# Attention in front of the feed forward, or in pieces between its products: a three-stage kernel on one core

## The chip, the core and the metric

The kernel runs on one core of a Trainium2 chip. The core has TensorE (PE, matrix products, with its weight loads as PEld), VectorE (DVE), ScalarE (ACT), GpSimd (POOL) and SyncE (SP, here only issuing DMAs). Each engine works off its own instructions in order; they meet only in semaphores. TensorE writes to PSUM (eight banks of 128 x 512 floats), the others read it from there and keep their results in SBUF. The metric is the device time of one execution in microseconds. A median of 3 runs of the kernel before is 901.97 us (901.59 to 902.38).

## The reference

```python
def _attn_ref(q, k, v):                  # (4, 8, 576, 64) each
    scores = scale * np.matmul(q, k.transpose(0, 1, 3, 2))
    mask = (rel >= 0) & (rel < 64)       # causal, a window of 64
    scores = np.where(mask, scores, -1000000000.0)
    attn = softmax(scores)               # max, exp, sum + 1e-9
    return np.matmul(attn, v)

def _moe_ref(x, w_in, w_out):            # x: 2304 x 512, w_in: 512 x 2048
    h = x @ w_in
    return (h - np.tanh(h)) @ w_out

def _moe2_ref(x, expert_emb, tau, w1, w2):
    # each row's best expert of 8 by cosine, its softmax weight as a gate;
    # out[mask] = gate * (np.maximum(x[mask] @ w1[e], 0) @ w2[e])
```

The three follow one another: attention's output, 2304 rows of 512, is the x of the feed forward, whose output is routed to the experts. All is float32. A product of the second and third stage is made of three products of "high" and "low" parts in a rounded type (float32r): high x high, high x low, low x high.

## The kernel before, in words

**Attention.** The sequence has 36 blocks of 64 positions (9 in each of 4 batches). A *group* is 3 such blocks of one pair of heads; there are 48 groups, each for one pair (4) and one *window* of 192 positions (12). Per group PE turns q and k (L1003, 3 transposes), DVE copies them out of PSUM (L721, L723: "evacuate"), PE makes the scores (L1012, 3 products in 6 records), DVE masks and takes the maximum (L728), ACT takes exp (L536), DVE inverts the sums (L749, L754), POOL scales (L416), PE turns the result (L1021), ACT copies it (L544), PE multiplies by v (L1032), ACT copies the output to xT (L553). DVE also copies v shifted by one block (L738). The engines run these steps skewed over the groups: in one round of PE stand transposes of group j, scores of j-1, turn of j-5 and attend of j-7. A hardware loop goes over the batches. POOL splits w_in meanwhile (L428, L431) from a staging buffer.

**Feed forward.** Only when all 48 groups are done does PE begin it. The rows are 6 blocks of 384 (two windows with all four pairs: 8 groups). A *step* (n, c) is one of 16 chunks of 128 hidden columns: `first_product(n, c)` (12 products of 384 columns), tanh on ACT (L581), h - tanh on DVE (L796), the high part on ACT (L585), the low part on DVE (L798), and, two steps later, `second_product` (9 products of 512 columns into three PSUM banks). PE's order is

```python
def step(n, c):
    first_product(n, c)
    if c >= 2:
        second_product(n, c - 2)
    ...
    if not (isinstance(n, int) and n == 0):
        after_block(n - 1, c)
```

where `after_block` routes the rows of the block before: transposes of x2 (L1097), logits (L1107), ranks, and small DVE work. In block 0 POOL splits w_out.

**Experts.** The rest, from the last product of the feed forward on, works through 25 tiles of rows with their expert's weights. The change doesn't touch it, only the buffers' places.

The order on every engine is written out by hand; SP issues the loads in the order of its own program, each waiting for the buffer that it fills.

Of the kernel before, what the change touches and what calls it, by code (L numbers as in the profile page):

```python
# [6 lines left out]
F32R = mybir.dt.float32r  # L7
# [4 lines left out]
ds = bass.ds  # L12
# [5 lines left out]
HEAD = 9  # L18
# [16 lines left out]
def build(nc, q, k, v, w_in, w_out, emb, tau, w1, w2, out):  # L35
# [15 lines left out]
    NT = T // P  # L51

# [9 lines left out]
    with ExitStack() as ctx:  # L62
# [37 lines left out]
        changes = sb("changes", [P, NTILE + 1])  # L100

        phase1 = ctx.enter_context(ExitStack())
        xT = sb("xT", [P, NW, PAIRS, GT], scope=phase1)
        win_h = sb("win_h", [P, KC, F], F32R, phase1)
        win_l = sb("win_l", [P, KC, F], F32R, phase1)
        attn = ExitStack()

        vw = [sb(f"vw{i}", [P, NB + 1, 2, D], scope=attn) for i in range(PAIRS)]
        qbd = [sb(f"qbd{i}", [P, NB, 2, WINDOW], scope=attn) for i in range(2)]
        sm = [sb(f"sm{i}", [P, GB, P], scope=attn) for i in range(4)]  # L110
        pn = [sb(f"pn{i}", [P, GB, P], scope=attn) for i in range(4)]
# [3 lines left out]
        plain_ones = sb("plain_ones", [P, P], scope=attn)  # L115
        plain_tri = sb("plain_tri", [P, P], scope=attn)
# [5 lines left out]
        stage = sb("stage", [P, 2, F], scope=attn)  # L122

        kT = [sb(f"kT{i}", [P, NB + 1, WINDOW], scope=attn) for i in range(2)]
        qk = [sb(f"qk{i}", [P, NB, 2, D], scope=attn) for i in range(2)]
        attn.close()
        wout_h = sb("wout_h", [P, FC, DM], F32R, phase1)
        wout_l = sb("wout_l", [P, FC, DM], F32R, phase1)
        xh = sb("xh", [P, KC, 2, 2, GT], F32R, phase1)
        xl = sb("xl", [P, KC, 2, 2, GT], F32R, phase1)  # L130
        early = ExitStack()
# [3 lines left out]
        zrow = sb("zrow", [1, DM], scope=early)  # L135
        en1 = sb("en1", [E, 3], scope=early)
        enroot = sb("enroot", [E, 1], scope=early)
        early.close()
        gf_tile = sb("gf", [P, 2, TB], scope=phase1)
        gf = [gf_tile[:, i, :] for i in range(2)]  # L140
        gh = [sb(f"gh{i}", [P, TB], F32R, phase1) for i in range(2)]
        gl = [sb(f"gl{i}", [P, TB], F32R, phase1) for i in range(2)]
# [3 lines left out]
        x2T, junk = (xT[:].rearrange("p w k t -> p (w k t)")[:, i * BANK:(i + 1) * BANK] for i in (0, 1))  # L146
# [38 lines left out]
        first_loaded, v_shifted = sem("first_loaded"), sem("v_shifted")  # L185
        qk_loaded, v_loaded = sems("qk_loaded", 2), sems("v_loaded", PAIRS)
        win_loaded, win_split = sem("win_loaded"), sem("win_split")
        win_high = sem("win_high")
        qk_transposed, qk_evacuated = sem("qk_transposed"), sem("qk_evacuated")
        scored, maxed, exped = sem("scored"), sem("maxed"), sem("exped")  # L190
        sum_padded, inverted, normed = sem("sum_padded"), sem("inverted"), sem("normed")
        p_transposed, pT_copied, attended, x_copied = sem("p_transposed"), sem("pT_copied"), sem("attended"), sem("x_copied")
        wout_loaded = sems("wout_loaded", ST)
# [28 lines left out]
        psT, psS, psP, psO = ([grouped(2 * n + i) for i in range(2)] for n in range(4))  # L222
        psH = [banks[:, i, 0:TB] for i in (0, 1)]
        acc = [banks[:, 2 + i, :] for i in range(ST)]
        psX = banks[:, 5, :]
        psX_last = [banks[:, i, :] for i in (5, 2, 3)]
        psJ = banks[:, 0, :]
        psL = banks[:, 6, 0:ST * E].rearrange("p (s e) -> p s e", s=ST)
        psR = banks[:, 7, 0:ST * E].rearrange("p (s e) -> p s e", s=ST)
        psN = banks[:, 7, 0:E]  # L230
# [15 lines left out]
        def attention(eng, step):  # L246

            for j in range(HEAD):
                step(0, j)
            with eng.Fori(0, B - 1) as b:  # L250
                for j in range(HEAD, HEAD + GPB):
                    step(b, j)
            for j in range(HEAD, GPB + 7):
                step(B - 1, j)

        def feed_forward(eng, step):

            for c in range(FC):
                step(0, c)
            with eng.Fori(1, NBLK - 1) as n:  # L260
                for c in range(FC):
                    step(n, c)
            for c in range(FC):
                step(NBLK - 1, c)
# [28 lines left out]

        block = ctx.enter_context(nc.Block())

        @block.sync
        def _(sp):
            def load_qk(b, hp):
                i = hp % 2

                wait(sp, qk_transposed, 0 if isinstance(b, int) and PAIRS * b + hp < 2 else GPB * b + GP * (hp - 1))
                for blocks, to in ((q_blocks, qk[i][0:WINDOW]), (k_blocks, qk[i][WINDOW:P])):
                    for h in range(2):
                        sp.dma_start(to[:, :, h, :], blocks[:, ds((2 * PAIRS * b + 2 * hp + h) * NB, NB), :]).then_inc(qk_loaded[i], 16)

            def load_v(b, hp):
                if not isinstance(b, int) or b > 0:

                    sp.wait_ge(attended, GPB * b + GP * (hp + 1 - PAIRS))
                for h in range(2):  # L310
                    sp.dma_start(vw[hp][0:WINDOW, 1:, h, :], v_blocks[:, ds((2 * PAIRS * b + 2 * hp + h) * NB, NB), :]).then_inc(v_loaded[hp], 16)

            def load_w_in(row):
                sp.dma_start(stage[:, ds(row % 2, 1), :], win_rows[:, ds(row, 1), :]).then_inc(win_loaded, 16)

            def load_batch(b, more=True):

                for hp in range(PAIRS):
                    load_v(b, hp)
# [958 lines left out]
```

## Time and profile before

| | |
|---|---|
| median of 3 runs | 901.97 us |
| span of the profiled execution, first to last instruction | 897.8 us |
| PE busy | 826.8 us (92%) |
| DVE busy | 431.8 us (48%) |
| ACT busy | 368.3 us (41%) |
| POOL busy | 188.9 us (21%) |

The profile gives the profiled execution's time as its span only; what lies around the span is the difference to the median, 901.97 - 897.8 = 4.2 us. Busy shares are means over three stages with different limits, so they have to be read stage by stage. The trace has one line per instruction or run of like instructions: start in us, length in us, engine, line, what is written from what, how often, and in brackets how long the engine had stood idle and who ended that.

### The profile page before, as it was taken

How to read it: one execution, taken by the hardware profiler on the slowest of the kernel's cores; microseconds unless marked ns; L12 is line 12 of the kernel's file. 1: busy time of each engine (PE TensorE's matmuls, PEld its weight loads, DVE VectorE, ACT ScalarE, POOL GpSimd, SP SyncE). 2: the span in 40 equal slices, each digit the busy share in tenths (PEclk: the TensorE clock that was granted, in tenths of full speed). 3: DMA queues.
4: the chain of work that ended last, by engine and by line, in shares of the span. 5: the costliest groups of instructions: out<-in, count | busy, mean ns of one | idle time of the engine just before them, and what ended most of it. 6: DMA issues, size and time to landing. Idle time of an engine off the chain costs nothing. (4 is left out here: it accounts for less than half of the span.)

```text
span 897.8 us, 16837 instructions
## 1 busy us (share of the span) xinstructions
PE 826.8 (92%) x4496; PEld 726.4 (81%) x4497; DVE 431.8 (48%) x1214; ACT 368.3 (41%) x888; POOL 188.9 (21%) x224
## 2 busy tenths in 40 slices
PE   5988878999999999999999999758999999999992
PEld 4877777999999999999999999637888888888871
DVE  6999996332343343344334334465435152355312
ACT  3888886233222223223223222506435262455423
POOL 3755557900001001001001001021111111111111
PEclk9999999999999999999999999869999999999996
DMA  9966841300000000000000320006634251655110
GB/s 166 185 147 142 133 92 36 118 1 32 5 1 1 35 0 0 35 0 0 35 0 0 128 95 1 36 25 223 224 120 141 79 193 41 224 216 212 64 36 25
DMA packets 80463, 72.87 MB, mean 81 GB/s; under 512 B 60364, under 2 KB 60497, under 8 KB 79906
## 3 DMA queue, kind: packets, MB, share of 16 engines
q1 hardware_dynamic: 75794, 61.00, 24.3%
q0 software_dynamic: 4624, 11.32, 3.9%
q8 instruction: 22, 0.36, 0.2%
q14 instruction: 23, 0.19, 0.1%
HBM read 138.19 MB, written 11.44 MB: 167 GB/s over the span
## 5 line engine op out<-in xcount | busy, mean ns | idle before, releaser
L1059 PE MATMUL banks<-xh,win_h 128*128 (+1 forms) x384 | 132.5, 345 | 0.0
L1061 PE MATMUL banks<-xh,win_l 128*128 (+1 forms) x384 | 129.4, 337 | 0.0
L1060 PE MATMUL banks<-xl,win_h 128*128 (+1 forms) x384 | 129.1, 336 | 0.0
L798 DVE TENSOR_TENSOR gl<-gf,gh 128x384 fp32r<-128x384 f32 x96 | 56.3, 587 | 145.2 <-ACT gh L585 145.2
L1061 PE MATMUL banks<-wout_h,gl 128*128 128x512 f32 x288 | 113.9, 395 | 0.0
L1060 PE MATMUL banks<-wout_l,gh 128*128 128x512 f32 x288 | 113.7, 395 | 0.0
L585 ACT CAST gh<-gf 128x384 fp32r<-128x384 f32 x96 | 49.3, 514 | 153.2 <-PE banks L1061 152.0
L1059 PE MATMUL banks<-wout_h,gh 128*128 128x512 f32 x288 | 112.2, 389 | 0.0
L796 DVE TENSOR_TENSOR gf<-banks,gf 128x384 f32<-128x384 f32 x96 | 53.4, 557 | 114.3 <-ACT gf L581 114.3
L581 ACT ACTIVATE gf<-banks 128x384 f32<-128x384 f32 x96 | 47.2, 492 | 148.3 <-PE banks L1061 148.3
L961 DVE TENSOR_TENSOR hTl<-banks,hTh 128x512 fp32r<-128x512 f32 x50 | 32.3, 686 | 92.4 <-ACT hTh L669 92.3
L1059 PEld LDWEIGHTS banks<-xh,win_h 128*128 128x128 f32 x384 | 72.2, 188 | 2.6
L1060 PEld LDWEIGHTS banks<-xl,win_h 128*128 128x128 f32 x384 | 72.2, 188 | 2.5
L1059 PE MATMUL banks<-w1h,xgh 128*128 x176 | 70.5, 400 | 2.7 <-DVE xgl L969 2.7
L1061 PEld LDWEIGHTS banks<-xh,win_l 128*128 128x128 f32 x384 | 72.0, 188 | 0.0
L1059 PE MATMUL banks<-w2h,hTh 128*128 x176 | 70.8, 402 | 0.9 <-DVE hTl L961 0.9
L536 ACT ACTIVATE sm<-sm,nmx 128x128 f32<-128x128 f32 x144 | 56.2, 391 | 33.5 <-DVE nmx L728 33.5
L1061 PE MATMUL banks<-w2h,hTl 128*128 x176 | 68.9, 392 | 0.0
L1061 PE MATMUL banks<-w1h,xgl 128*128 x176 | 68.8, 391 | 0.0
L1060 PE MATMUL banks<-w1l,xgh 128*128 x176 | 68.7, 390 | 0.0
L1060 PE MATMUL banks<-w2l,hTh 128*128 x176 | 68.6, 390 | 0.0
L484 POOL TENSOR_TENSOR norm<-ss,power 128x3 f32<-128x3 f32 x6 | 5.3, 884 | 297.5 <-DVE ss L819 281.0
(181 smaller groups left out, 1532.0 us busy)
## 6 DMA issues: line engine op xcount, KB each, us to landing
w1raw<-in_moe_w_dram SPq DMA_DIRECT2D x104, 512.0 KB
w2raw<-in_moe_w_dram SPq DMA_DIRECT2D x104, 512.0 KB
vw<-in_v_dram SPq DMA_DIRECT2D x32, 144.0 KB, 4.0
x_rows<-x SPq DMA_DIRECT2D x6, 768.0 KB, 3.6
qk<-in_q_dram SPq DMA_DIRECT2D x30, 144.0 KB, 3.2
qk<-in_k_dram SPq DMA_DIRECT2D x30, 144.0 KB, 3.6
stage<-in_moe_w_in_dram SPq DMA_DIRECT2D x4, 1024.0 KB, 6.4
x<-in_moe_w_out_dram SPq DMA_DIRECT2D x16, 256.0 KB, 2.6
```

What stands on the lines that cost most here:

```text
L484: pool.tensor_tensor(norm[:], ss[:], power[:], ALU.pow).then_inc(rooted, 1)
L536: last = act.activation(sm[j % 4][:, u, :], sm[j % 4][:, u, :], ACT.Exp, bias=nmx[:, j % 4, u:u + 1], scale=-1.0, accum_out=rs[:, j % 4, u ...
L581: act.activation(gf[c % 2][:], psH[c % 2], ACT.Tanh).then_inc(tanh_ready, 1)
L585: act.copy(gh[c % 2][:], gf[c % 2][:]).then_inc(g_high, 1)
L796: dve.tensor_tensor(gf[c % 2][:], psH[c % 2], gf[c % 2][:], ALU.subtract).then_inc(g_ready, 1)
L798: dve.tensor_tensor(gl[c % 2][:], gf[c % 2][:], gh[c % 2][:], ALU.subtract).then_inc(g_split, 1)
L961: dve.tensor_tensor(hTl[:, part, :], psHT[half].rearrange("p (k t) -> p k t", k=KC), hTh[:, part, :], ALU.subtract).then_inc(hT_split, 1)
L1059: pe.matmul(to, sh, mh, start=start, stop=False)
L1060: pe.matmul(to, sh, ml, start=False, stop=False)
L1061: return pe.matmul(to, sl, mh, start=False, stop=stop)
```

## The change

Only the 8 groups of block 0 stand in front of the feed forward. The other 40 groups are cut into pieces (transposes, score, turn, attend on PE, and their counterparts on the others), and each piece stands in a *slot*. A step has two slots: 2c behind its first product, 2c+1 behind its second product. The groups of block 1 begin every 3 slots from slot 0 of block 0; those of block n begin every 4 slots, from 8 slots ahead of block n-1. A group's score stands 1 slot behind its beginning, exp 2, inversion and scaling 3, turn 6, attend and its copy 7, the split of x 8. In the slots one PSUM bank (5) holds both a group's transposes and scores, one (6) both its turned weights and its output; routing moves to bank 7 with x2 turned in halves.

Other edits: v is loaded twice, once per half of the partitions, in place of DVE's shifted copy; the last block of keys of a window is carried to the next by a small DVE copy (L803); POOL scales in place; w_in and w_out are loaded whole and their low part is written over the raw one, w_in by POOL one chunk of 128 columns per step of block 0, w_out by ACT and DVE; x is split by POOL group by group instead of by ACT and DVE; there are no hardware loops over batches and blocks any more; constants are made at other places.

```diff
-HEAD = 9
+LAG_SCORE, LAG_TURN, LAG_ATTEND = 1, 6, 7
+    FIRST, SLOTS = 2 * PAIRS, 2 * FC
+    WIN_COLS = (0, 2 * P, BANK, 2 * BANK, 3 * BANK, F)
...
+        def first_slot(g):
+            n, i = g // FIRST - 1, g % FIRST
+            return 3 * i if n == 0 else SLOTS * n + 4 * i - 8
+        begins = {first_slot(g): g for g in range(FIRST, NG)}
+        def begun(s, lag):
+            return begins.get(s - lag)
...
 # PE
+            def pieces(s):
+                if (g := begun(s, LAG_ATTEND)) is not None:
+                    attend(g)
+                if (g := begun(s, LAG_TURN)) is not None:
+                    transpose_p(g)
+                if (g := begun(s, LAG_SCORE)) is not None:
+                    score(g)
+                if (g := begun(s, 0)) is not None:
+                    transpose_qk(g)
...
+            for n in range(NBLK):
+                for c, s in steps(n):
+                    first_product(n, c)
+                    pieces(s)
+                    if c >= 2:
+                        second_product(n, c - 2)
+                    elif n > 0:
+                        second_product(n - 1, c + FC - 2)
+                    pieces(s + 1)
+                    if n > 0:
+                        route(n - 1, c)
...
 # DVE
+            def evacuate(g):
...
+                if window_of(g) % GP:
+                    carries[0] += 1
+                    dve.tensor_copy(kT[hp][:, 0, :], kT[hp][:, GB, :]).then_inc(carried, 1)
+                    dve.wait_ge(carried, carries[0])
+                dve.tensor_copy(kT[hp][:, 1:1 + GB, :], psT(g)[:, :, WINDOW:P]).then_inc(qk_evacuated, 1)
...
+                    less_tanh(n, c)
+                    pieces(s)
...
+                    low_g(n, c)
+                    pieces(s + 1)
...
 # ACT
+                    tanh(n, c)
+                    pieces(s)
+                    high_g(n, c)
+                    pieces(s + 1)
+                    if n == 0:
+                        high_w_out(c)
...
 # POOL
+                    if n == 0 and c + 2 < FC:
+                        split_w_in(c + 2)
+                    pieces(s)
+                    pieces(s + 1)
```

Three places show the order. The first is PE around the end of the attention in front. `qk`, `pn` and `sm` are q with k, the scaled weights and the weights scaled in place; `xh`, `win_h` mark the first product. Before:

```order
L1021 MATMUL banks<-ident,pn 128x128 x3
L1032 MATMUL banks<-pT,vw 128x128 x9
L1052 MATMUL banks<-ident,embn 128x8 x4
L1059 MATMUL banks<-xh,win_h 128x384
L1060 MATMUL banks<-xl,win_h 128x384
L1061 MATMUL banks<-xh,win_l 128x384
```

And now, behind the first first product (12 such rows, the last two of which are shown):

```order
L1163 MATMUL banks<-xl,win_h 128x384
L1164 MATMUL banks<-xh,win_l 128x384
L1103 MATMUL banks<-ident,qk 128x128 x3
L1112 MATMUL banks<-kT,qbd 128x128 x3
L1162 MATMUL banks<-xh,win_h 128x384
```

The transposes of group 8 and its scores stand directly behind one another, with no product between them. The second place is PE in a step with a turn and an attend; before, the last rows of a first product and the beginning of a second one:

```order
L1059 MATMUL banks<-xh,win_h 128x384
L1060 MATMUL banks<-xl,win_h 128x384
L1061 MATMUL banks<-xh,win_l 128x384
L1059 MATMUL banks<-wout_h,gh 128x512
L1060 MATMUL banks<-wout_l,gh 128x512
```

Now, in block 0 (the nine rows of the second product are cut to its ends by the two fences):

```order
L1123 MATMUL banks<-ident,sm 128x128 x3
L1103 MATMUL banks<-ident,qk 128x128 x3
L1162 MATMUL banks<-wout_h,gh 128x512
L1163 MATMUL banks<-wout_l,gh 128x512
L1164 MATMUL banks<-wout_h,gl 128x512
```

```order
L1164 MATMUL banks<-wout_h,gl 128x512
L1135 MATMUL banks<-pT,vw 128x128 x3
L1112 MATMUL banks<-kT,qbd 128x128 x3
L1162 MATMUL banks<-xh,win_h 128x384
L1163 MATMUL banks<-xl,win_h 128x384
```

Turn and attend of one group, and transposes and score of the next, are parted by one second product. The third place is DVE in a later block, one step with an evacuation and the beginning of the next. L870 is h - tanh, L874 the low part of g, L799 to L805 the evacuation with its carried keys, L810 mask and maximum; before, only L796, L798 and the small routing work stood here:

```order
L870 TENSOR_TENSOR gf<-banks,gf 128x384
L799 TENSOR_SCALAR qbd<-banks 64x3x64 x2
L803 COPY kT<-kT 128x64
L805 COPY kT<-banks 128x192
L874 TENSOR_TENSOR gl<-gf,gh 128x384
L810 ISA sm,nmx<-banks,mask 128x128
L810 ISA nmx 128x1
```

The evacuation has moved behind h - tanh of the same step. The last is SP ahead of the first feed forward product: four loads of v for groups 4 and 5, one of w_out, eight of q and k for groups 8 and 9 (cut where a batch ends), then four of v for groups 6 and 7.

```order
L356 DMA vw<-in_v_dram 64x6x64
L358 DMA vw<-in_v_dram 64x5x64
L356 DMA vw<-in_v_dram 64x6x64
L358 DMA vw<-in_v_dram 64x5x64
L366 DMA wout_raw<-in_moe_w_out_dram 128x4x512
L349 DMA qk<-in_q_dram 64x3x64 x2
L349 DMA qk<-in_k_dram 64x3x64 x2
L349 DMA qk<-in_q_dram 64x3x64 x2
L349 DMA qk<-in_k_dram 64x3x64 x2
L356 DMA vw<-in_v_dram 64x6x64
L358 DMA vw<-in_v_dram 64x5x64
```

Before, one load of a whole pair and batch (64x9x64) stood where several smaller ones stand now.

## Rows read from the trace of the kernel before

**Rows 1.** Windows: length, busy PE PEld DVE ACT POOL, clock, DMA share, GB/s.

```profile
0.00:42.70 42.70, 29.98 (x209) 27.96 (x211) 34.62 (x162) 24.24 (x100) 22.19 (x48) 0.96 0.97 175
42.70:148.30 105.60, 83.89 (x662) 74.30 (x660) 100.98 (x434) 87.66 (x340) 58.22 (x70) 1.00 0.56 113
148.30:572.80 424.50, 424.46 (x2218) 385.47 (x2217) 156.99 (x378) 113.42 (x231) 52.26 (x52) 1.00 0.08 28
572.80:897.80 325.00, 288.47 (x1412) 238.66 (x1412) 139.16 (x241) 142.94 (x219) 56.26 (x55) 0.94 0.37 128
...
20.00:25.00 5.00, 4.59 (x27) 4.59 (x28) 3.89 (x20) 2.26 (x10) 2.61 (x3) 0.66 1.36 182
```

**Rows 2.** Timeline of PE, attention: a round without a wait, then a waited score.

```profile
27.43 0.49 PE L1003 MATMUL banks<-ident,qk 128*128 128x128 f32 x3
27.76 0.83 PE L1012 MATMUL banks<-kT,qbd 128*128 128x128 f32 x6
28.43 0.49 PE L1021 MATMUL banks<-ident,pn 128*128 128x128 f32 x3
28.75 0.83 PE L1032 MATMUL banks<-pT,vw 128*128 128x128 f32 x6
29.43 0.49 PE L1003 MATMUL banks<-ident,qk 128*128 128x128 f32 x3
...
126.39 0.94 PE L1012 MATMUL banks<-kT,qbd 128*128 128x128 f32 x6 [0.48 <-DVE kT L723]
127.16 0.49 PE L1021 MATMUL banks<-ident,pn 128*128 128x128 f32 x3
```

**Rows 3.** Timeline of PE, feed forward: second product, x2 transposes, first product.

```profile
225.85 0.39 PE L1059 MATMUL banks<-wout_h,gh 128*128 128x512 f32 x1
...
227.93 0.60 PE L1097 MATMUL banks<-ident,x 128*128 128x128 f32 x4
228.29 0.42 PE L1059 MATMUL banks<-xh,win_h 128*128 x1
228.55 0.33 PE L1060 MATMUL banks<-xl,win_h 128*128 x1
...
230.47 0.39 PE L1059 MATMUL banks<-wout_h,gh 128*128 128x512 f32 x1
```

**Rows 4.** Timeline, head: PE's loads waited for; an SP issue.

```profile
0.77 1.41 SPq L332 DMA_DIRECT2D qk<-in_q_dram  x2
...
20.41 0.55 PE L1003 MATMUL banks<-ident,qk 128*128 128x128 f32 x3 [2.66 <-DMA qk<-in_k_dram]
...
26.76 0.83 PE L1032 MATMUL banks<-pT,vw 128*128 128x128 f32 x6
```

**Rows 5.** DMA issues by line: KB each, us from issue to landing.

```profile
qk<-in_k_dram SPq DMA_DIRECT2D x2, 96.0 KB, 2.8
```

**Rows 6.** Timeline of DVE and ACT: tanh in a step; evacuation; exp and copy.

```profile
226.05 0.49 ACT L581 ACTIVATE gf<-banks 128x384 f32<-128x384 f32 x1 [1.54 <-PE banks L1061]
226.58 0.56 DVE L796 TENSOR_TENSOR gf<-banks,gf 128x384 f32<-128x384 f32 x1 [1.47 <-ACT gf L581]
...
42.26 0.72 DVE L721 TENSOR_SCALAR qbd<-banks 64x192 f32<-64x192 f32 x2
43.00 0.36 DVE L723 COPY kT<-banks 128x192 f32<-128x192 f32 x1
...
25.50 0.40 ACT L536 ACTIVATE sm<-sm,nmx 128x128 f32<-128x128 f32 x1 [0.99 <-DVE nmx L728]
...
26.66 0.46 ACT L544 COPY pT<-banks 128x384 f32<-128x384 f32 x1
```

**Rows 7.** Timeline of DVE and POOL: a short fill; a split beside a DVE operation.

```profile
1.41 0.11 DVE L709 MEMSET kT<- 128x64 f32 x1
...
45.15 1.27 POOL L431 TENSOR_TENSOR win_l<-stage,win_h 128x512 fp32r<-128x512 f32 x1
45.55 0.90 DVE L749 TENSOR_SCALAR rse<-rs 128x3 f32<-128x3 f32 x1
```

More of the change, by code:

```diff
@@ L292, in chained, with steps @@
             return then
+        def steps(n):
+            for c in range(FC):
+                yield c, SLOTS * n + 2 * c
         block = ctx.enter_context(nc.Block())
@@ L297, in _ @@
         def _(sp):
[L298 to L302, printed above, removed]
-                    for h in range(2):
[L304 to L319, printed above, removed]
-                    if hp + 2 < PAIRS or more:
-                        load_qk(b + (hp + 2) // PAIRS, (hp + 2) % PAIRS)
-                    if hp == 1 and more:
-                        sp.wait_ge(win_high, 4 * b + 1)
-                        wait(sp, win_split, 4 * b)
-                        load_w_in(b + 1)
@@ new lines, in load_qk @@
+            def load_qk(u, only=None):
+                wait(sp, qk_transposed, 2 * u - 2)
+                for w, start, end in parts(u):
+                    if only is not None:
+                        start, end = only
+                    for blocks, to in ((q_blocks, qk[u % 2][0:WINDOW]), (k_blocks, qk[u % 2][WINDOW:P])):
+                        for h in range(2):
+                            at = (2 * PAIRS * (w // GP) + 2 * (u % PAIRS) + h) * NB + GB * (w % GP) + (start if only else 0)
+                            loaded = first_loaded if only and start == 0 else qk_loaded[u % 2]
+                            sp.dma_start(to[:, start:end, h, :], blocks[:, at:at + end - start, :]).then_inc(loaded, 16)
@@ L1006, in score, with loads @@
-            def score(b, j):
-                g = GPB * b + j
-                i, first = j // GP % 2, j % GP * GB
-                pe.wait_ge(qk_evacuated, g + 1)
-                wait(pe, maxed, g - 1)
-                for u in range(first, first + GB):
-                    last = pe.matmul(psS[j % 2][:, u - first, :], qbd[i][:, u, :, :].rearrange("p h c -> p (h c)"), kT[i][:, u:u + 2, :],
+            def loads(u, each):
+                n = sum(each * (1 if v // PAIRS % GP != 1 else 2) for v in range(u % 2, u + 1, 2))
+                return 16 * n
```

781 lines of the change are left out of this document (424 added, 357 removed).

## The prediction

> **What bounds the kernel now.** I read the windows by stage first, since a mean over stages says nothing here [rows 1]. Up to 148.3 us is attention: from 42.7 on DVE is busy 100.98 of 105.6 us and PE 83.89. From 148.3 to 572.8 is the feed forward: PE is busy 424.46 of 424.50 us, DVE 157, ACT 113. The last 325.0 us are routing's end and the experts. So attention goes at DVE's pace with PE partly idle, and the feed forward at PE's with the others mostly idle. The timeline of PE then shows why: in attention a score waits 0.48 us for DVE's evacuation, while a round without a wait takes 29.43 - 27.43 = 2.00 us [rows 2]. In the feed forward the products follow each other without a gap: a second product takes 227.93 - 225.85 = 2.08 us, a first one 12 x (230.47 - 228.55)/11 = 2.09 us [rows 3].
>
> **What can be won.** 40 groups leave the front. What they cost there is the time between the end of group 7 and 148.3; what they cost inside is PE's time for them, since PE has no gap to hide them in, plus whatever waits arise. The sum is over PE's path: start of the feed forward, its length, and the 325.0 us behind it, which I leave as they are (no line of the experts changes; their first weights are asked for in block 4 as before).
>
> **Start of the feed forward.** PE's order ahead of it is 13 rounds. Up to group 1's attend I take the trace of before: there the second attend starts at 26.76 and lasts 0.67, so 27.4, behind a wait of PE for q and k at 20.41 [rows 4]. Now PE waits first for q and k of groups 4 and 5, the 22nd to 25th load at 0.68 us each and 2.8 us to land: 19.5 or 20, which I count as equal. Then SP decides: its load of v for groups 4 and 5 waits for the attends of groups 0 and 1, and behind it stand, in order, 4 + 1 + 8 + 4 = 17 issues until v for groups 6 and 7 is asked for. An issue takes 1.41/2 = 0.70 us in the row; with 0.68 that is 11.5 us, so the last ends at 38.9 or 39. A 96 KB load lands 2.8 us from its issue's start [rows 5]: 38.3 + 2.8 = 41.1. The other engines are not that late: PE has about 5 us without work by then. In the trace a wait of 2.66 us at 20.41 goes with a granted clock of 0.66 in the window of 20 to 25, that is about 3.4 us at 1.2 instead of 2.4 GHz [rows 1, 4]. So the two attends left take 2 x 1.34 = 2.7 us, to 43.9. Then ACT's copy and POOL's split of x in two operations on 192 columns, which the trace does not show; ACT's copy of 384 columns takes 0.46 [rows 6], POOL's subtraction of 512 takes 1.27 [rows 7]. Bounds 1.0 and 3.5 us, I take 1.9. The first product starts at about 46 (43 to 50), against 148.3: **-102.3 us**.
>
> **The pieces on PE.** A group's transposes, scores, turn and attend took 2.00 us in a round without a wait [rows 2]. Is anything added by changing between them and the rounded products? The four x2 transposes say no: from 227.93 to 228.29 are 0.36 us, and the first product behind them gives back 228.55 - 228.29 = 0.26 instead of 0.17, so 0.45 for 4, 0.11 each [rows 3], as in attention (18 records x 0.112 = 2.0). 40 x 2.02 = **+80.7 us**.
>
> **New waits inside.** A piece follows the one that it needs after one product, and the engines between have that long. Let T be the end of a first product.
> - Evacuation before score: PE is back at T + 0.33 + 2.08 = T + 2.41. DVE: h - tanh starts at T + 0.73 (226.58 - 225.85) and takes 0.56; the evacuation takes 43.36 - 42.26 = 1.10; a wake-up about 0.05: T + 2.44 [rows 3, 6]. The carried keys add a copy of 64 columns and a wait on itself: the nearest rows are 0.11 for a fill of that shape [rows 7] and 0.36 for 192 columns [rows 6]; I take 0.17: T + 2.61. Of the 32 groups of blocks 2 to 5, all of which begin behind a first product, 24 carry. A score that waits costs 0.77 instead of 0.67 besides (127.16 - 126.39, [rows 2]). By these ends 24 x 0.30 + 8 x 0.13 = 8.2 us; if DVE's operations overlap by the 0.09 us that successive rows often show, nearly nothing. I take 24 x 0.2 + 8 x 0.05 = **+5.2 us**. In block 0 the turn and the attend stand before the score, which leaves 1 us more, so nothing there.
> - Turn before attend: ACT's tanh starts at T + 0.20 and takes 0.49, exp up to the copy 26.66 - 25.50 = 1.16, the copy 0.46: T + 2.31, against T + 2.41. Nothing, by a margin of 0.1; if it is missed, 0.2 x 32 = 6 us [rows 6].
> - Slot 0: score 8 stands right behind its transposes, so PE waits from T + 0.33 to about T + 2.6: **+2.2 us**.
> - The clock: PE idle before the first product leaves its first microseconds at 1.2 GHz; by the 3.4 us of above half is lost: **+2 us** (0 to 4).
> - The transposes of the embedding (0.4 us) now stand inside: **+0.4 us**.
> - Loads in block 0. SP's program runs on from 38.9: between it and q and k for groups 12 and 13 stand 35 issues (24 us), then their own 8 (5.4), so they land by 71. They are due in slot 12: 46 + 6 steps of 4.2 + pieces and the wait, about 80. The margin is 9 us, so nothing; but all of it is in one queue with 7.3 MB of weights.
> - POOL's split of w_in: two operations, the dearer of 1.27 us [rows 7], at most 2.5 us per chunk plus about 1.2 for the groups, of a step of 5.4,, and it begins two steps ahead. Hidden. ACT and DVE likewise: DVE's 101/38 = 2.7 us a group at most [rows 1] in one and a half steps, beside some 1.8 us a step. If this cover went, it would be PE waiting for a chunk.
> - What goes from ACT and DVE (x split, shifted v) lay beside PE in the feed forward: nothing.
>
> **Sum.** -102.3 + 80.7 + 5.2 + 2.2 + 2 + 0.4 = -11.8 us, on a span of 897.8: 886.0. The time around the span (4.2 us) stays: 901.97 - 11.8 = **890 us**.
>
> **Two rules weighed.** Beside a running split of POOL (45.15 to 46.42) an operation of DVE on three columns lasts 0.90 us, and ends when POOL's does [rows 7]. The Trainium skill (GPSIMD Engine Reference, Specifications) says that GpSimd's SBUF interfaces are shared with VectorE, with contention for two-input or two-port DVE operations; the trace agrees. By that rule the low parts, which have two SBUF inputs, would be held up beside POOL's splits in block 0: this is rival C, and the sum would be the one there instead of the one above.
>
> The Trainium skill (DMA: Bandwidth & Descriptors, Specifications) asks for transfers of at least 512 B for line rate, and the change reads v a second time in rows of 256 B, which speaks against it. The trace has 175 GB/s in the head, made mostly of such rows [rows 1], more than the 98 KB per 0.68 us = 144 GB/s that SP issues; by the rule the loads and not the issues would set the head, and the sum would move towards rival B.
>
> **Rivals.**
> A. *Every hand-over is late* (slower). The four hand-overs of a group (transposes, evacuate, score; turn, copy, attend) have margins of 0.1 us or less by my count, while DVE and ACT have one more waiting operation each in front, and choosing and placing of the routing (small DVE operations) in steps 10 and 12. If evacuation and copy come 0.35 us later each than PE needs them, a group costs 0.7 us: 36 x 0.7 = 25 instead of 5 us, so -11.8 + 20 = +8: 910. It decides from (11.8 + 5.2)/36 = 0.47 us a group on. For it: the margins. Against: the durations are read, not guessed, and a late piece doesn't delay the next.
> B. *q and k of group 12 come late.* SP is in order, its waits and 43 issues from 39 us on; should an issue stretch to 0.95 us, a third more than the row has, in a full queue, that is 43 x 0.27 = 12 us later, against a margin of 9, and the head by 17 x 0.27 = 5 us: 890 + 5 + 3 = 898, up to 905.
> C. *DVE beside POOL.* A two-input operation held 0.7 us in each of the 16 steps of block 0, of which PE sees at most half: +6, 896.
> D. *Less waiting than counted*: overlap takes the 5.2 and the clock's 2, the head starts at 43: 880.
>
> **Chances.** Forecast (884 to 896) 0.45; A 0.25; B 0.12; C 0.08; D 0.10. About 0.2%, 1.8 us, is what a measurement tells from no change. Faster: forecast, D, C, most of B, 0.68. Slower: most of A, a little of B, 0.24. Same: 0.08. The range takes D's end and A's value: 880 to 910. The forecast's own is 884 to 896.
>
> **What would show it.** In the new profile: the first xh product near 46 us; between it and the experts 514 or 515 us (424.5 + 80.7 + waits) with PE busy all but some 10 us; PE's transposes, scores, turns and attends at 0.11 us each record when they don't wait; waits of PE on kT in blocks 2 to 5 of 0.1 to 0.2 us each and none on pT; a wait of 2.2 us at the first slot; none on qk's DMA in block 0; 325 us from the last second product to the end. The prediction is wrong if the head passes 50 us, if PE waits more than 0.45 us per group, or if the experts' stage is not the same.

## The result, and the profile after

The changed kernel takes 891.72 us (median of 4 runs, 890.83 to 894.78), the kernel before beside it 902.17 (4 runs, 901.59 to 903.31): ratio 0.9891, 95% interval 0.9869 to 0.9914, or 10.4 us less. The profiled execution is the slowest of the four: 894.78 us with a span of 893.0, where the other three have spans of 889.1 to 890.1.

The windows of the changed kernel, cut at its first product and behind its last second product, and a short one (columns as in [rows 1]):

```profile
0.00:49.10 49.10, 26.80 (x144) 23.73 (x145) 18.58 (x101) 19.59 (x74) 22.31 (x52) 0.83 0.55 134
49.10:566.40 517.30, 513.78 (x2940) 463.00 (x2940) 240.44 (x863) 199.84 (x587) 123.16 (x183) 0.99 0.22 56
566.40:893.00 326.60, 290.84 (x1412) 240.37 (x1412) 139.25 (x241) 142.90 (x219) 56.19 (x55) 0.94 0.37 128
50.00:55.00 5.00, 3.74 (x14) 3.41 (x12) 1.05 (x3) 0.96 (x3) 2.85 (x3) 0.67 1.10 286
```

Against [rows 1] the front is 99.1 us shorter (49.2 for 148.3), the feed forward with the pieces in it 92.8 us longer (517.3 for 424.5), the rest 1.6 us longer (326.6 for 325.0). PE is busy 513.78 of 517.30 us; DVE, which was busy 100.98 of 105.6 us in attention, is busy 46% of the long stretch. The bound is now PE nearly everywhere, and what 105.6 us of attention at DVE's pace held in idle PE (105.6 - 83.89 = 21.7 us) is what was to be won. Less than that came out. Part of it stands in the front again: its 49.10 us hold 22.3 us of idle PE, and the first 42.7 us of the kernel before held 12.7 [rows 1]. The low clock and the late scores below are the other parts.

PE's waits in the changed kernel (engine, line, releaser: us in total, times, longest), first up to 50 us (0.8 us for copies of pT left out), then, of those from 44 to 565 us, what stands behind the first product:

```profile
PE banks L1103 <- DMA qk<-in_k_dram: 13.6, 4, 5.6
PE banks L1123 <- POOL sm L472: 3.7, 5, 1.5
PE banks L1135 <- DMA vw<-in_v_dram: 2.4, 1, 2.4
PE banks L1162 <- POOL xl L482: 1.8, 1, 1.8
```

```profile
PE banks L1112 <- DVE kT L805: 3.4, 2, 2.0
```

After the first product there are two waits with a name, both for an evacuation and both in the first slots. That is not all that PE loses, as the timeline shows. First the end of the front and the first slots (PE; first, middle and last parts of a product left out):

```profile
44.46 2.90 PE L1135 MATMUL banks<-pT,vw 128*128 128x128 f32 x12 [2.40 <-DMA vw<-in_v_dram]
49.17 0.69 PE L1162 MATMUL banks<-xh,win_h 128*128 128x384 f32 x1 [1.80 <-POOL xl L482]
50.29 0.53 PE L1162 MATMUL banks<-xh,win_h 128*128 128x384 f32 x1
...
53.17 0.57 PE L1103 MATMUL banks<-ident,qk 128*128 128x128 f32 x3
55.78 0.94 PE L1112 MATMUL banks<-kT,qbd 128*128 128x128 f32 x6 [2.04 <-DVE kT L805]
56.47 0.44 PE L1162 MATMUL banks<-xh,win_h 128*128 128x384 f32 x1
56.73 0.50 PE L1163 MATMUL banks<-xl,win_h 128*128 128x384 f32 x1
57.03 0.52 PE L1164 MATMUL banks<-xh,win_l 128*128 128x384 f32 x1
...
60.20 0.49 PE L1103 MATMUL banks<-ident,qk 128*128 128x128 f32 x3
...
64.09 0.94 PE L1112 MATMUL banks<-kT,qbd 128*128 128x128 f32 x6 [1.31 <-DVE kT L805]
```

The first product takes 53.17 - 49.17 = 4.00 us and the second 60.20 - 56.47 = 3.73, where 2.09 is the length at 2.4 GHz [rows 3]: most of both went at 1.2 GHz, which cost 1.9 + 1.6 = 3.5 us. The clock was not low all the way. The score at 55.78 took 0.94 us for its six records, as the waited one in [rows 2], and the second product's first record 0.44; from 57.03 on the records take 0.52 us again. So the clock had risen by the end of the wait of 2.04 us, and behind that wait it fell a second time. Group 8's score waits 2.04 us at slot 0, and the second group's 1.31 at 64.09, which stands behind a first product only.

Then a score of a group that carries keys (group 25, of block 3, which begins in the last steps of block 1), on PE and on DVE. No wait is printed, yet the score starts 0.40 us behind the last product's start where the products follow at 0.23:

```profile
221.35 0.39 PE L1163 MATMUL banks<-wout_l,gh 128*128 128x512 f32 x1
221.57 0.39 PE L1164 MATMUL banks<-wout_h,gl 128*128 128x512 f32 x1
221.97 0.94 PE L1112 MATMUL banks<-kT,qbd 128*128 128x128 f32 x6
222.66 0.42 PE L1162 MATMUL banks<-xh,win_h 128*128 128x384 f32 x1
```

```profile
220.12 0.56 DVE L870 TENSOR_TENSOR gf<-banks,gf 128x384 f32<-128x384 f32 x1 [1.86 <-ACT gf L652]
220.60 0.71 DVE L799 TENSOR_SCALAR qbd<-banks 64x192 f32<-64x192 f32 x2
221.32 0.20 DVE L803 COPY kT<-kT 128x64 f32<-128x64 f32 x1
221.55 0.36 DVE L805 COPY kT<-banks 128x192 f32<-128x192 f32 x1
```

The last copy ends at 221.91, the score starts at 221.97: it waited, and the page books the wait as busy time, since a matmul's end is modelled to run on into the gap. The starts of the first products tell it apart: a step takes 5.17 us with turn and attend in it, 5.22 with a score that carries nothing, 5.45 with one that carries (steps without routing work).

### The profile page after: what moved, and what is told of

Read it like the earlier page. It is cut to its first block and busy times, and to the rows that moved or that the text cites. A ratio compares the mean times of both kernels' runs of the same rounds, so it can differ in the third digit from the quotient of the medians.

```text
span 893.0 us, 16016 instructions
## 1 busy us (share of the span) xinstructions
PE 831.4 (93%) x4496; PEld 727.1 (81%) x4497; DVE 398.3 (45%) x1205; ACT 362.3 (41%) x880; POOL 201.7 (23%) x288
## 3 DMA queue, kind: packets, MB, share of 16 engines
q1 hardware_dynamic: 96610, 65.20, 24.7%
## 5 line engine op out<-in xcount | busy, mean ns | idle before, releaser
L1162 PE MATMUL banks<-xh,win_h 128*128 128x384 f32 x384 | 137.4, 358 | 1.8 <-POOL xl L482 1.8
L1164 PE MATMUL banks<-xh,win_l 128*128 128x384 f32 x384 | 130.8, 341 | 0.0
L1163 PE MATMUL banks<-xl,win_h 128*128 128x384 f32 x384 | 130.4, 340 | 0.0
L870 DVE TENSOR_TENSOR gf<-banks,gf 128x384 f32<-128x384 f32 x96 | 53.5, 557 | 157.3 <-ACT gf L652 157.3
L1162 PE MATMUL banks<-wout_h,gh 128*128 128x512 f32 x288 | 119.1, 414 | 0.0
L472 POOL TENSOR_TENSOR sm<-sm,rr 128x384 f32<-128x384 f32 x48 | 41.9, 874 | 305.7 <-DVE rr L821 305.7
L874 DVE TENSOR_TENSOR gl<-gf,gh 128x384 fp32r<-128x384 f32 x96 | 55.1, 574 | 112.7 <-ACT gh L659 108.1
L659 ACT CAST gh<-gf 128x384 fp32r<-128x384 f32 x96 | 49.2, 512 | 128.9 <-PE banks L1164 127.7
```

The lines of the kernel that those rows point to most:

```text
L472: pool.tensor_tensor(sm[g % 4][:], sm[g % 4][:], rr[:, g % 4, :].unsqueeze(2).broadcast_to((P, GB, P)), ALU.mult).then_inc(normed, 1)
L659: act.copy(gh[c % 2][:], gf[c % 2][:]).then_inc(g_high, 1)
L870: dve.tensor_tensor(gf[c % 2][:], psH[c % 2], gf[c % 2][:], ALU.subtract).then_inc(g_ready, 1)
L874: dve.tensor_tensor(gl[c % 2][:], gf[c % 2][:], gh[c % 2][:], ALU.subtract).then_inc(g_split, 1)
L1162: pe.matmul(to, sh, mh, start=start, stop=False)
L1163: pe.matmul(to, sh, ml, start=False, stop=False)
```

## The experiments

Theory: the changed kernel runs at PE's pace, so that whatever PE waits for or has too much of shows in the time one to one; it pays at DVE's copy of the carried keys, at the first slots, and at the front's loads. Rival: the parts beside PE (DVE, loads) are close behind it, so that taking one wait away only brings the next. "Before" is the median of the kernel before on the same chip; the chips differ a little, so kernels are compared with each other by their ratios.

**e1_carry_early: the carried keys' copy moved ahead.** DVE copies them before h - tanh (or before the low part) rather than inside the evacuation.

```diff
+                    carry(begun(s, 0))
                     less_tanh(n, c)
                     pieces(s)
...
-                    dve.tensor_copy(kT[hp][:, 0, :], kT[hp][:, GB, :]).then_inc(carried, 1)
```

> The copy of the carried keys is moved ahead of h - tanh (or of the low part) of its step; nothing else. Theory 1 (PE waits in the score steps because DVE's evacuation with the carried copy ends about 0.2 us after PE is back): steps with a carrying group fall from 5.46 to about 5.2 us, 24 groups x 0.27 = 6.5 us, 891.7 -> 885 to 886. Rival (the 5.46 us steps come from the change between kinds of products on PE or from the bank that transposes and scores share): the steps keep their length, within 1 us of 891.7. Rival 2 (the copy is late for another reason, ACT's tanh): half of it, 888.

883.75 us (5 runs; before 900.42), ratio 0.981 [0.9787, 0.9832], 7 us under the changed kernel. In the trace DVE's copy is at 212.61 and the score of the same group follows its product at the pace of products:

```profile
215.98 0.40 PE L1174 MATMUL banks<-wout_h,gl 128*128 128x512 f32 x1
216.21 0.86 PE L1122 MATMUL banks<-kT,qbd 128*128 128x128 f32 x6
216.83 0.42 PE L1172 MATMUL banks<-xh,win_h 128*128 128x384 f32 x1
```

From the last part to the next product: 0.85 us, and 222.66 - 221.57 = 1.09 in the changed kernel. The steps with a carrying group that took 5.45 now take 5.23; there are 22 of them, since the other two of the 24 begin in block 0, where an attend stands between their transposes and their score and nothing changed. The starts of blocks 1 and 5 are 346.8 us apart against 352.0, so 5.2 us are the carry. The two profiled executions are 11.3 us apart in span, and the other 6 are not the edit's: the front, whose program is the same, ends 2.0 us sooner (47.15 for 49.17); the first step of block 0 takes 5.40 for 7.30, because its product went at 2.4 GHz this time (2.21 us for 4.00; the clock fell behind the wait at slot 0, and the second product took 3.60); and what follows block 5's start is 1.9 us shorter.

**e2_turn_twice: a double turn.** Inside, every group's three transposes of the softmax are made twice.

```diff
+                if g >= FIRST:
+                    for u in range(GB):
+                        last = pe.transpose(psP(g)[:, u, :], sm[g % 4][:, u, :], ident[:])
```

> Each of the 40 groups inside the feed forward turns its weights twice (3 more transposes of 128x128 a group, the same result). Theory 1 (PE is the bound there and pays 0.11 us for each such record, wherever it stands): 120 x 0.112 = 13.4 us more, 905. Rival (pieces fill gaps in which PE would wait anyway): under 4 us more. Rival 2 (a piece costs more than its records, for the change of kind): over 20 us more, 912.

902.87 us (10 runs), ratio 1.0025 [1.001, 1.0039]: 12 us over the changed kernel by the ratios, from 120 small transposes, or 0.1 us each; in the traces the starts of blocks 0 and 5 are 453.7 us apart for 441.6. The steps with a turn went from 5.17 to 5.49. PE has no slack for even 0.32 us a group: in the products the pieces are paid in full.

**e3_loads_order: the front's loads in another order.**

```diff
-            load_v(2)
             load_wout(0)
             load_qk(4)
+            load_v(2)
             load_v(3)
```

> Only SP's order in the head is changed: w_out's first part and q, k of groups 8 and 9 are asked for ahead of v of groups 4 and 5, in the time in which SP waits for the second attend. Theory 1 (the head's end hangs on v of groups 6 and 7, which stands behind these 9 issues): v is asked for 4 us earlier and the first product starts at about 45 instead of 49.2 us; 891.7 -> 887 to 888. Rival (POOL's scaling behind its splits, and ACT, set the head's end by then): 1 us or less. Rival 2 (more loads in flight delay v of groups 4 and 5): no change or up to 2 us slower.

888.55 us (4 runs), ratio 0.9863 [0.9838, 0.9888]. The last two attends stand at 41.27 without a wait for v, and the first product at 45.45 instead of 49.17 (47.15 and 48.44 in e1 and e2, whose front has the changed kernel's program):

```profile
41.27 2.09 PE L1135 MATMUL banks<-pT,vw 128*128 128x128 f32 x12
45.45 0.44 PE L1162 MATMUL banks<-xh,win_h 128*128 128x384 f32 x1 [2.09 <-POOL xl L482]
```

The intervals of the two kernels overlap by a little, so the 2.5 us rest on the trace as much as on the ratio, and there on 1.7 to 3.7 us of the front.

**e4_v_twice_alone: one part of the change by itself.** The kernel before, with v read twice by DMA and without DVE's shifted copy; nothing interleaved.

```diff
+  sp.dma_start(vw[hp][WINDOW:P, 0:NB, h, :], v_blocks[:, ds(..., NB), :]).then_inc(v_loaded[hp], 16)
...
-                    shift_v(b, j - 5)
```

> The kernel before with one part of the change alone: v is loaded twice, and DVE's shifted copy (48 x 0.81 us) is gone; attention still stands whole in front. Theory 1 (attention in front goes at DVE's pace, 2.75 us a round, the next engine is ACT at about 2.4 us): 40 rounds x 0.35 = 14 us, 902 -> 888, so as much as the whole change brings. Rival (SP's 12 issues of 0.65 us for each 3 groups, 2.6 us a round, or the loads of 256 B rows, become the bound): 5 to 7 us, 896. Rival 2 (the shift was hidden): no change.

892.84 us (6 runs), ratio 0.9904 [0.9883, 0.9926]. The feed forward begins at 142.33, 6.0 us sooner. Not theory 1's 888: rounds of 2.0 us do appear, but they are broken by loads, which the kernel before did not wait for in attention. PE's waits from 42.7 to 148.3 us, first of this kernel, then of the kernel before:

```profile
PE banks L1002 <- DMA qk<-in_k_dram: 8.0, 6, 3.1
PE banks L1020 <- ACT pT L545: 2.0, 3, 0.9
```

```profile
PE banks L1012 <- DVE kT L723: 17.3, 33, 1.3
PE banks L1021 <- ACT pT L544: 2.2, 3, 1.3
```

17.3 us of waiting for DVE are gone and 8.0 us for loads have come. The rest is the clock:

```profile
42.70:142.30 99.60, 87.39 (x684) 81.11 (x683) 72.16 (x405) 89.92 (x348) 56.44 (x73) 0.95 0.91 162
```

PE is busy 87.39 us where it was 83.89 [rows 1], at a granted clock of 0.95 for 1.00. So 17.3 - 8.0 - 3.5 = 5.8 of the 6.0 us. So one edit of a few lines nearly matches the whole rebuilding (0.9904 and 0.9891, not to be told apart). That left two readings of the changed kernel, which e10 tells apart.

**e10_v_shift_inside: that part undone in the changed kernel.** Only one block of 64 positions per load is read twice, DVE copies the rest.

```diff
-                        sp.dma_start(vw[u % 2][0:WINDOW, start + skip:end, h, :],
-                                     v_blocks[:, at - 1 + skip:at + end - start - 1, :]).then_inc(v_loaded[u % 2], 16)
+                        one = start + skip
+                        sp.dma_start(vw[u % 2][0:WINDOW, one:one + 1, h, :],
+                                     v_blocks[:, at - 1 + skip:at + skip, :]).then_inc(v_loaded[u % 2], 16)
...
+                    last = dve.tensor_copy(vw[u % 2][0:WINDOW, first:end], vw[u % 2][WINDOW:P, first - 1:end - 1])
```

> Changed kernel without the second read of v: only one block of 64 positions per load is read a second time, the other rows are copied from the first by DVE, one operation per load of two groups, as the kernel before copies them. As many issues of SP, fewer packets, 20 to 24 more operations on DVE. Theory 1 (between the products DVE has room, so the second read is worth nothing there, and the whole gain of the change could be had by the interleaving alone): 890 to 892, ratio 0.988 to 0.990, 1 us of it less through the head's loads or 1 us more through a DVE operation ahead of a score. Theory 2 (what the second read brought alone, 0.9904 in the kernel before, is part of what the changed kernel gains, because DVE is close behind PE there too): 895 to 900, ratio 0.993 to 0.998.

891.23 us (6 runs; before 901.95), ratio 0.9878 [0.9858, 0.9899]: the same as the changed kernel. The group of DVE's new copies (count, busy us, mean ns, then the idle time ahead of them):

```profile
L831 DVE COPY vw<-vw 64x512 f32<-64x512 f32 (+3 forms) x32 | 14.6, 478 | 7.9 <-DMA vw<-in_v_dram 7.2
```

Of these 14.6 us, 10.6 lie in the long stretch (DVE is busy 251.05 us there for 240.44), and it lasts as long as before, 516.6 us from the first product to the last part of the second ones for 516.8. In the front PE waits 2.1 us for such a copy where it waited 2.4 us for the load. So DVE's work cost nothing between the products, and the two parts are two ways to the same idle time of PE and do not add: relieve DVE in attention, or put attention where DVE has room.

**e5_slot0: the first transposes earlier.** Group 8's transposes stand ahead of the first product, its evacuation ahead of the first h - tanh.

```diff
+                    if s == 0:
+                        pieces(s)
                     first_product(n, c)
-                    pieces(s)
+                    if s:
+                        pieces(s)
```

> Changed kernel with group 8's transposes before the first product and its evacuation before the first low part. In the changed kernel PE waits 2.04 us for that evacuation at 55.78, right behind the transposes. Theory 1 (the wait is a hole in PE's work): it goes, so 889 to 890, 2 us under the changed kernel's 891.7 or ratio 0.987. Theory 2 (what PE does not wait at slot 0 it gives back to the clock, which is at 1.2 GHz there and rises at a set amount of work, or to slot 4): ratio 0.989 as the changed kernel.

887.29 us (4 runs; before 901.21), ratio 0.9851 [0.9833, 0.9868]. The score at slot 0 follows its product without a wait, and the second product is already quick (53.08 to 53.62 to 54.15: 0.53 us for three parts, where three take 0.96 at 1.2 GHz):

```profile
51.11 0.52 PE L1165 MATMUL banks<-xh,win_h 128*128 128x384 f32 x1
51.89 0.83 PE L1115 MATMUL banks<-kT,qbd 128*128 128x128 f32 x6
52.48 0.42 PE L1165 MATMUL banks<-xh,win_h 128*128 128x384 f32 x1
53.08 0.34 PE L1165 MATMUL banks<-xh,win_h 128*128 128x384 f32 x1
```

Block 0 takes 85.2 instead of 89.6 us. The 2.04 us are gone, 0.4 of the second wait (0.92 for 1.31), and the other 1.6 to 2 us are the clock, which no theory had counted as a gain: with the wait there, the second product had gone at 1.2 GHz again. The first product still took 3.8 us.

**e6_warm: PE kept busy in the front.** Transposes of the identity that nobody reads: 10 ahead of each of two turns, 28 ahead of the last attends, 16 ahead of the first product.

```diff
+                if j in (FIRST + 1, FIRST + 2):
+                    warm_array(10)
...
+                if j == FIRST + 3:
+                    warm_array(28)
...
+            warm_array(16)
```

> Changed kernel with transposes of the identity that nobody reads put into PE's order in the gaps of the head (10 ahead of each of two turns, 28 ahead of an attend, 16 ahead of the first product). In the changed kernel PE is granted 1.2 GHz from about 40 to 60 us and the first two steps take 6.6 and 7.3 instead of 5.2 and 5.3 us. Theory 1 (the idle PE before the first product is why the clock is low): the clock is full by the first product, 3.5 us are won there and up to 1.5 in the last attends: 887 to 888, ratio 0.984. Theory 2 (the clock rises only with the products themselves, or the extra transposes hold up the turns behind them): 891 to 893, ratio 0.989 to 0.991.

889.03 us (4 runs), ratio 0.9867 [0.9851, 0.9883]: between the theories, and hardly apart from the changed kernel's interval. The trace is clearer. The granted clock is full where it was 0.50, and the first product takes 2.2 us:

```profile
40.00:45.00 5.00, 4.47 (x42) 4.29 (x41) 0.00 (x0) 1.58 (x4) 2.31 (x4) 1.00 0.64 152
45.00:50.00 5.00, 4.65 (x37) 4.41 (x36) 0.00 (x0) 1.25 (x4) 3.31 (x6) 1.00 1.03 298
```

The first product's 2.2 us alone prove little, since e1's took as long without these transposes. But there the clock fell behind the wait at slot 0, and here it does not, though the wait is as long:

```profile
53.28 0.94 PE L1112 MATMUL banks<-kT,qbd 128*128 128x128 f32 x6 [2.08 <-DVE kT L805]
53.97 0.42 PE L1171 MATMUL banks<-xh,win_h 128*128 128x384 f32 x1
54.23 0.34 PE L1172 MATMUL banks<-xl,win_h 128*128 128x384 f32 x1
```

In the three traces with such transposes (e6, e9, e11) the clock is full from 40 us to the end of block 0; in the seven others of the changed kernel and its variants it is low for a part of that time. Block 0 takes 86.3 us for 89.6. The start is hardly sooner (48.48 for 49.17).

**e8_four: four moves at once.** Those of e1, e3 and e5, and POOL's order in the front: the splits of x two rounds later, w_in's first chunk at round 10, so that no split stands ahead of a normalising that PE waits for. Of the edit only this fourth part is shown.

```diff
-                if j in (4, 5):
-                    split_w_in(j - 4)
-                if 5 <= j:
-                    split_x(j - 5)
+                if j == FIRST + 2:
+                    split_w_in(0)
+                if 7 <= j:
+                    split_x(j - 7)
...
+                    if s == 0:
+                        split_w_in(1)
```

> Changed kernel with four things moved at once and nothing added: the carried keys' copy early (883.8 alone, 0.981), wout(0) and q and k of groups 4 and 5 asked for ahead of v(2) (888.6 alone, 0.9863), group 8's transposes and evacuation early (2 us by the wait that it shows), and POOL's normalising in the head ahead of its splits (PE waits 3.7 us for it in five places). Theory 1 (the four are separate holes of PE): -6 -3 -2 -1 from 891.7 is 879 to 880, ratio 0.976. Theory 2 (the head is one chain, so that the parts in it overlap, and in the first steps the clock takes back what waits give): 882, ratio 0.979.

878.13 us (5 runs; before 901.21), ratio 0.9744 [0.9725, 0.9762]. By themselves e1, e3 and e5 brought 0.0081, 0.0028 and 0.0040 against the changed kernel's 0.9891, 0.0149 in all; together with the fourth 0.0147. Within the intervals (0.002 to 0.0025 either way, each) they add up, as separate holes of PE should, and the trace has them: 5.3 us less in blocks 1 to 4, 4.6 less in block 0, a front 5.1 shorter. What the fourth brought is not to be told: the ratios leave nothing for it, and the front's end, 1.4 us ahead of e3's, is within what fronts of the same program differed by (2.0 us). PE's waits for normalising are gone, but 2.4 us of waits for copies of pT stand where 0.8 did, and POOL's put-off splits now end the front, and PE waits 3.3 us for the last of them:

```profile
40.26 0.49 PE L1118 MATMUL banks<-ident,qk 128*128 128x128 f32 x3
44.07 0.44 PE L1177 MATMUL banks<-xh,win_h 128*128 128x384 f32 x1 [3.32 <-POOL xl L482]
```

**e9_five** is e8 with e6's transposes.

> The four moves of the run before this one, and the transposes of the identity in the head's gaps. Theory 1 (the low clock costs by itself): 3 to 4 us less than with the four: 876, ratio 0.971. Theory 2 (with the waits gone the clock is full anyway, or the extra transposes now stand in the way): same as the four or 1 us more, 880, ratio 0.976.

877.31 us (5 runs), ratio 0.9738 [0.9724, 0.9752]: as e8. The clock is full (block 0 takes 83.7 us for 85.0), but the first product is later, 45.52 for 44.07, since the 28 transposes put the last attends from 38.84 to 41.92. The trace shows both, 1.45 us lost and 1.3 won.

**e11_warm_behind** is e8 with 28 such transposes only behind the last attend, where PE waits anyway.

```diff
+            for kk in range(28):
+                pe.transpose(banks[:, 1, 0:P], ident[:], ident[:])
```

> The four moves (878.1, ratio 0.9744, or 13.3 us under the changed kernel) and 28 transposes of the identity only behind the last attend, where PE waits 3.32 us for POOL's split of x anyway, and none ahead of it, where in the run with five edits they put the last attend from 38.84 to 41.92. Theory 1 (an idle PE is what lowers the clock in the first two steps, 1.5 to 2 us, and the five edits gave it back by the later attend): first product at 44 with the clock full, 876.5, ratio 0.9725. Theory 2 (the clock isn't won by work so late, or the start moves): 878, ratio 0.974 to 0.975.

876.99 us (5 runs; before 901.95), ratio 0.9725 [0.9704, 0.9746]. By ratio this is not to be told from e8 or e9; in the trace the first product is at 44.36 and block 0 takes 83.6 us. It is the fastest kernel of this study, 2.75% under the kernel before and 1.7% under the changed one. Its windows:

```profile
0.00:44.36 44.36, 27.66 (x176) 25.27 (x177) 18.29 (x103) 19.48 (x74) 20.31 (x50) 1.00 0.61 150
44.36:550.50 506.14, 504.83 (x2937) 459.38 (x2937) 241.72 (x862) 199.98 (x587) 125.14 (x184) 1.00 0.22 57
550.50:875.20 324.70, 288.40 (x1413) 238.78 (x1412) 139.36 (x241) 142.84 (x220) 56.16 (x55) 0.94 0.37 128
```

506.1 - 424.5 = 81.6 us for what stands inside. 1.0 of it is the wait that is left at slot 4, 0.3 one for DVE's maxima, and 0.4 the embedding's transposes, so some 79.9 us are PE's work for the 40 groups, 2.0 each. (The 1.00 for the clock of the front doesn't hold in its early part: a score at 21.20 takes 1.49 us, as at 1.2 GHz.)

## Why the prediction was right, and where its terms were off

It held: faster, with 891.7 where 890 stood, and no rival came. But the nearness flatters the sum. The sum was for the profiled execution, and there it reads, against -11.8 forecast:

| term | forecast | measured | from |
|---|---|---|---|
| front | -102.3 | -99.1 | 49.17 against 148.3 |
| pieces on PE | +80.7 | +80.7 | as forecast; e11 gives 79.9 |
| waits at first slots | +2.2 | +3.4 | 2.04 + 1.31 |
| clock at the start | +2 | +3.5 | two products of 4.00 and 3.73 us |
| evacuation before score | +5.2 | +4.8 | what is left of 92.8; e1 by itself: 5.2 |
| embedding | +0.4 | +0.4 | inside, not measured apart |
| behind the last second product | 0 | +1.6 | 326.6 against 325.0 |
| sum | -11.8 | -4.7 | spans 893.0 and 897.8: -4.8 |

The two terms without a measurement of their own, pieces and embedding, stand as forecast and one is the remainder, so the sum has to come out; e1 and e11 are what checks it, to about 1 us.

Against the spans the forecast is 7 us off: 886.0 stood for a span that was 893.0. The two spans stand 4.8 us apart, the medians 10.4. The step that failed here is "the time around the span (4.2 us) stays". In every execution with both numbers the time is 1.7 to 1.9 us over the span (894.78 and 893.0; 883.49 and 881.7). So the profiled execution of the kernel before, with its span of 897.8, took about 899.6 us by this rule, 2.4 less than its median: I took a quick execution for the typical one. That of the changed kernel is 3.1 us above its median. A sum of terms against one execution carries such differences, and mine was lucky in them. What the other executions of the changed kernel did better is not in any trace. But the traces of e1 and e2, with the same program up to the first product, start it at 47.15 and 48.44, so the front was worth 99.9 to 101.2 us in them, nearer to the forecast of 102.3; e1's first step was 1.9 us shorter, nearly all of it by the clock; and the part behind the last second product took 323.6 to 328.0 us over all traces (from the start of its last record), with no line of the experts changed, so the 1.6 us in the table are no effect of the change.

- **The front** (46 forecast, 49.2 measured) went wrong at its first number. I took attend 1 from the trace of before, 27.4 us [rows 4]; it was done at 29.97 and SP's load behind it issued at 30.16. What I had of the chain behind that held: the last of v's issues ended at 42.4, 12.3 us later, against 11.5. The 0.8 us are mostly one pair of issues of q that took 2.38 us where the others took 1.3. The 2.6 us at the front's first number have two grounds. PE waited 5.61 us for q and k, not 2.66, up to 20.79 instead of 20.41, and then worked at 1.2 GHz up to 26.0 (a score 1.49 us), where the kernel before did from some 21.3 to 24.7. And DVE's carried keys stood in the evacuation beside POOL's split of w_in, here in POOL's and DVE's rows:

```profile
25.01 1.27 POOL L491 TENSOR_TENSOR win_l<-win_raw,win_h 128x512 fp32r<-128x512 f32 x1
```

```profile
25.57 0.76 DVE L803 COPY kT<-kT 128x64 f32<-128x64 f32 x1 [0.56 <-PE banks L1112]
```

A copy that takes 0.20 took 0.76 and ended with POOL's operation; the maxima, ACT's exp behind them and the copy of pT that stands behind exp in ACT's order all came after it, and attend 1 waited 0.60 us for that copy. I had costed the splits by their place on POOL, not by what they do to DVE in the front. e3 shows that v's place in SP's queue was worth 1.7 to 3.7 us of the front.
- **The pieces** were right, 2.0 us each in e11 for 2.02. That changing between transposes in float32 and rounded products costs nothing was read from one row and holds: in e1 a step with two products alone takes 4.19 us, one with turn and attend 5.17, one with transposes and score 5.22, so 0.98 + 1.03 = 2.01 a group.
- **Evacuation before score** was right in place, sign and size (22 waits of about 0.23 for the carried keys, e1, where 24 of 0.2 were counted). It was also right that turn before attend has room: 5.17 a step.
- **The first slots.** The wait at slot 0 was forecast as 2.2 and is 2.04. The one at slot 4 was missed. "The turn and the attend stand before the score" is true in block 0 only from the third group inside on; the second has just one first product between its transposes and its score (60.20 to 64.09), since step 1 has no second product yet.
- **The clock** cost 3.5 and not 2. I had scaled from another wait and counted one low stretch; there were two, and the second stands behind the wait at slot 0. Without that wait it is not there (e5).
- **Loads in block 0, ACT and DVE's other work**: nothing, as forecast. PE waits for no DMA behind the first product.
- **Rival C** had its mechanism right and its price wrong. In block 0 the low parts (L874) take 662 ns in the mean of 15, and 557 in blocks 1 to 4 without splits; single ones take 0.9 us. That is 0.1 us each where I had put 0.7, and PE did not wait for it. In the front, where I had not looked for it, it is the 0.76 above. The Trainium skill's rule (GPSIMD Engine Reference, Specifications) had named two-input or two-port DVE operations; the trace agrees on the low parts. The copy held up has one input, so the rule covers it only if it is one of the two-port operations, which no trace here shows.
- **Rival B's ground**, that loads and not issues set the pace, came in another kernel: with v read twice and nothing between the groups (e4), PE waits 8.0 us for loads, at 190 GB/s from 42.7 to 100 us, most of it in rows of 256 B (79308 of that kernel's 99407 packets are under 512 B). That the size of the rows is the reason was not tested. In the changed kernel PE waits for no load behind the first product.
- **Not asked** was whether the two parts of the change are one gain or two. I priced the second read of v at nothing in the new place, rightly, but did not see that in the old place it would have brought 8.6 us at once.

## What to carry to other kernels

Before work is moved under a busy engine, ask what the same idle time would cost to win where it is: here a few lines brought 0.96% and the rebuilding 1.1%. Small moves then took the rebuilding to 2.75%; whether moves of that kind would have taken the few lines' kernel as far was not run. Once the bound engine is one engine throughout, the terms add up, and the remaining money is in small hand-overs: put the operations that don't depend on the late input (a carry, a first transpose) in front of it. Price a front by what is queued behind each moved operation, and fill an idle PE just before its long stretch only where it waits anyway (here 1 us, seen in the trace alone).

## What the runs showed of the hardware

- Waits of 0.2 us of PE between full products don't appear in the view of waits: busy time of PE was 513.78 of 517.30 us while some 5 us of late scores were in it. Distances between the starts of products show them: equal steps agree to 0.04 us.
- A wait can cost more than its length: behind one of 2.04 us the clock fell and the second product took 3.73 us for 2.09. Taking the wait away brought 4 us (e5). It need not fall: in e6 it stayed up behind a wait of 2.08 us.
- Beside POOL's subtraction of 512 columns (1.27 us) a DVE copy of 64 columns lasted 0.76 instead of 0.20 us and ended with it.
- The clock at the first product differs between executions of one program: 4.00 us for it in the changed kernel's trace and 2.21 in e1's, whose program is the same up to there. With small transposes in the idle time ahead of it (28 of them, 3.1 us, in e11) it was at 2.4 GHz from the first record on and stayed there to the end of block 0, in all three such kernels; in the seven without them it was low for some time.
- Executions of one kernel lay up to 5 us apart (889.52 to 894.64 in six runs of e10), more than some of the effects looked for. Where two kernels differed by under 3 us the lengths of steps in the traces told them apart; a front's length, which differed by 2.0 us with one program, did so only beyond that.
